# Alpha, key and query loaded as runs of three tokens, identity products in place of transposes, and POOL's order at gate piece 2

## What is computed

```python
# 1: gated linear attention; state starts at zero
for t in range(S):
    state = alpha[:, :, t, :, None] * state + einsum('bhd,bhe->bhde', k[:, :, t], v[:, :, t])
    y[:, :, t] = einsum('bhd,bhde->bhe', q[:, :, t], state)
x = y.transpose(0, 2, 1, 3).reshape(B * S, H * D)
# 2: normalised gated network, d_ff = 1536
xn = x / sqrt(mean(x * x, -1) + 1e-6) * rms_g
x = (silu(xn @ w_gate) * (xn @ w_val)) @ w_out
# 3: four experts of width 1024, weighted by normalised probabilities p
out = sum(p[:, e:e+1] * (relu(x @ w1[e]) @ w2[e]) for e in range(4))
```

## Time and profile before

| | us |
|---|---|
| median of 3 runs | 703.69 (703.68 to 704.35) |
| the profiled execution's own time | 704.28 |
| its span, first to last instruction | 702.2 |
| PE busy in it | 687.1 (98%) |
| DVE busy | 460.6 (66%) |
| POOL busy | 320.3 (46%) |
| ACT busy | 259.9 (37%) |

### The profile page before, as it was taken

How to read it: one execution, slowest core, us unless ns; L and a number is a source line. 1 busy time by engine, 2 the same in 40 slices (tenths; PEclk the granted TensorE clock), 3 DMA queues, 4 the chain that set the end, 5 groups by cost and what they waited for, 6 DMA issues and landing times.

```text
span 702.2 us, 10687 instructions
## 1 busy us (share of the span) xinstructions
PE 687.1 (98%) x3998; PEld 636.4 (91%) x3998; DVE 460.6 (66%) x808; ACT 259.9 (37%) x472; POOL 320.3 (46%) x401
## 2 busy tenths in 40 slices
PE   7889999999999999999999999999999999999998
PEld 6679999999999999998899999999999999999997
DVE  6975656655545633315848777877787779777876
ACT  3931234222522243226413344434343434443430
POOL 3467771111111124840294685558555865577200
PEclk9999999999999999999999999999999999999999
DMA  8994380005102000200001101110111001100003
GB/s 180 225 180 111 84 174 14 7 4 103 35 1 77 1 1 24 68 0 1 1 22 47 46 1 45 46 46 4 42 46 46 23 23 46 45 24 1 22 1 135
DMA packets 71749, 35.13 MB, mean 50 GB/s; under 512 B 53905, under 2 KB 70673, under 8 KB 71697
## 3 DMA queue, kind: packets, MB, share of 16 engines
q1 hardware_dynamic: 71696, 34.44, 19.5%
HBM read 31.48 MB, written 2.36 MB: 48 GB/s over the span
## 4 chain that ended last, share of the span: by engine, by line
PE 90%; SPq 6%; DVE 2%; issue 1%; POOL 1%; DMA 1%; ACT 0%; DVEq 0%
PE out_ps L1339 13%; PE out_ps L1341 13%; PE out_ps L1340 13%; PE hid_ps L1332 7%; PE hid_ps L1334 7%; PE hid_ps L1333 7%; PE at_ps L1544 4%; PE at_ps L1543 4%; PE at_ps L1542 4%; SPq L453 3%; PE hid_ps L1543 2%; PE hid_ps L1544 2%; PE hid_ps L1542 2%; PE at_ps L1382 2%; PE at_ps L1396 1%; PE at_ps L1428 1%
## 5 line engine op out<-in xcount | busy, mean ns | idle before, releaser
L1214 DVE SCALAR_TENSOR_TENSOR x<-out_ps,prob,x 128x384 f32<-128x384 f32 x180 | 110.3, 613 | 58.7 <-PE out_ps L1341 58.7
L1339 PE MATMUL out_ps<-early_r,late_r 128*128 128x384 f32 x384 | 129.1, 336 | 0.3 <-DVE x L1214 0.3
L1340 PE MATMUL out_ps<-early_r,late_r 128*128 128x384 f32 x384 | 129.4, 337 | 0.0
L1341 PE MATMUL out_ps<-early_r,late_r 128*128 128x384 f32 x384 | 129.3, 337 | 0.0
L669 POOL TENSOR_TENSOR hid_lo<-act_sb,hid_hi 128x384 fp32r<-128x384 f32 x44 | 45.0, 1022 | 170.3 <-ACT hid_hi L857 170.3
L913 ACT COPY late<-at_ps 128x512 f32<-128x512 f32 x98 | 57.7, 589 | 108.0 <-PE at_ps L1544 105.2
L1179 DVE TENSOR_TENSOR act_sb<-hid_ps,act_sb 128x384 f32<-128x384 f32 x48 | 26.6, 554 | 80.5 <-PE hid_ps L1334 71.1
L1339 PEld LDWEIGHTS out_ps<-early_r,late_r 128*128 128x128 f32 x384 | 72.1, 188 | 6.6 <-DVE x L1214 0.9
L1340 PEld LDWEIGHTS out_ps<-early_r,late_r 128*128 128x128 f32 x384 | 72.0, 188 | 5.3
L1341 PEld LDWEIGHTS out_ps<-early_r,late_r 128*128 128x128 f32 x384 | 72.1, 188 | 0.0
L723 POOL TENSOR_TENSOR early<-stage 128x128 f32<-128x128 f32 x14 | 6.5, 467 | 129.4 <-PE at_ps L1544 102.5
(11 more groups left out here) (272 smaller groups left out, 1614.5 us busy)
## 6 DMA issues: line engine op xcount, KB each, us to landing
stage<-in_moe_w_dram SPq DMA_DIRECT2D x32, 384.0 KB, 3.3
alpha_all<-in_alpha_dram SPq DMA_DIRECT2D x8, 288.0 KB, 6.1
stage<-in_moe_w_out_dram SPq DMA_DIRECT2D x4, 576.0 KB, 4.1
out_dram<-x SPq DMA_DIRECT2D x12, 192.0 KB, 1.9
stage<-in_moe_w_gate_dram SPq DMA_DIRECT2D x8, 216.0 KB, 4.1
stage<-in_moe_w_val_dram SPq DMA_DIRECT2D x8, 216.0 KB, 4.0
a_tm<-in_alpha_dram SPq DMA_DIRECT2D x9, 192.0 KB, 3.8
k_tm<-in_k_dram SPq DMA_DIRECT2D x9, 192.0 KB, 4.0
```

Of the source, the lines that this page charges most:

```text
L1214: dve.scalar_tensor_tensor(out=a, in0=part, scalar=p, in1=a, op0=ALU.mult, op1=ALU.add).then_inc(s_acc, 1)
L1339: pe.matmul(dst, ah, bh, start=first, stop=False)
L1340: pe.matmul(dst, ah, bl, start=False, stop=False)
L1341: return pe.matmul(dst, al, bh, start=False, stop=last)
```

## The change

The three tiles become [128, 8, 160]: a head's 160 columns are three tokens of 48 and one hole of 16 behind them. Partition p holds tokens 3p, 3p + 1 and 3p + 2, so a run in DRAM is 144 numbers, 576 bytes, and one DMA loads what three did. PE turns each head and token slot with one float32 product with the identity (64 columns of the head as the weights, 48 of the slot and 16 of what follows, the identity as the moving operand), whose 128 results go to every third column of the bank: 6 products for a tensor of a pair in place of 3 transposes. The semaphore counts follow (16 in place of 48), the clamp and the hole fill run over the smaller tiles. The value tensor keeps its three DMAs. On POOL, `hidden_lo(1)` moves from behind `split(3)` to a place inside it, after the rounding (L596) and before the wait for it and the subtractions.

```diff
+    HEAD = NCH * D + HOLE
-        q_tm = sb("q_tm", [P, NCH, H * LANE], stack=reg_a)
-        k_tm = sb("k_tm", [P, NCH, H * LANE], stack=reg_a)
-        a_tm = sb("a_tm", [P, NCH, H * LANE], stack=reg_a)
+        q_tm = sb("q_tm", [P, H, HEAD], stack=reg_a)
+        k_tm = sb("k_tm", [P, H, HEAD], stack=reg_a)
+        a_tm = sb("a_tm", [P, H, HEAD], stack=reg_a)
...
-                for c in range(NCH):
-                    sp.dma_start(dst[:, c, :].rearrange("p (h x) -> p h x", h=H)[:, hs, 0:D],
-                                 src[b, hs, t0 + c * CH:t0 + (c + 1) * CH, :].rearrange("h p d -> p h d")
-                                 ).then_inc(arrived or done, 16)
+                if which < 3:
+                    sp.dma_start(dst[:, hs, 0:NCH * D],
+                                 src[b, hs, t0:t0 + TQ, :].rearrange("h (p c) d -> p h (c d)", c=NCH)
+                                 ).then_inc(arrived or done, 16)
+                    return
...
-        def split(pool, n):
+        def split(pool, n, between=None):
...
             pool.tensor_scalar(hi, stage_view(n % 2, *shape), 0.0, 1.0, ALU.add, ALU.mult).then_inc(s_whi, 1)
+            if between:
+                between()
             pool.wait_ge(s_whi, n + 1)
...
-                make(pool.memset(t[:, :, :].rearrange("p c (h x) -> p (c h) x", h=H)[:, :, D:LANE], 1.0))
+                make(pool.memset(t[:, :, NCH * D:HEAD], 1.0))
...
-                    if f < FT - 1:
+                    if f < FT - 1 and FT * i + f != 1:
                         hidden_lo(FT * i + f)
                     if i == 0 and f < NPIECE - EARLY:
-                        split(pool, EARLY + f)
+                        split(pool, EARLY + f, None if f else lambda: hidden_lo(1))
...
-                        part = a_tm[:, :, 0:H // 2 * LANE] if f else a_tm[:, :, H // 2 * LANE:]
+                        part = a_tm[:, 0:H // 2, :] if f else a_tm[:, H // 2:, :]
...
                         for c in range(NCH):
-                            mm = pe.transpose(banks[bank][:, c * CH:(c + 1) * CH],
-                                              tm[:, c, n * 2 * LANE:(n + 1) * 2 * LANE], ident[:, :])
+                            for a in range(2):
+                                mm = pe.matmul(banks[bank][a * LANE:(a + 1) * LANE, bass.ds(c, CH, step=NCH)],
+                                               tm[:, 2 * n + a, c * D:c * D + LANE], ident[:, :], start=True,
+                                               stop=True)
```

More of the change, by code:

```diff
@@ L450, in load_quarter @@
                 hs = slice(first_head, last_head)
-                src, dst, done = ((alpha, a_tm, s_qka[0]), (k, k_tm, s_qka[1]), (q, q_tm, s_qka[2]), (v, v_tm, s_v))[which]
+                if which < 3:
+                    src, dst, done = ((alpha, a_tm, s_qka[0]), (k, k_tm, s_qka[1]), (q, q_tm, s_qka[2]))[which]
+                    sp.dma_start(dst[:, hs, 0:NCH * D],
+                                 src[b, hs, t0:t0 + TQ, :].rearrange("h (p c) d -> p h (c d)", c=NCH)
+                                 ).then_inc(arrived or done, 16)
+                    return
                 for c in range(NCH):
-                    sp.dma_start(dst[:, c, :].rearrange("p (h x) -> p h x", h=H)[:, hs, 0:D],
-                                 src[b, hs, t0 + c * CH:t0 + (c + 1) * CH, :].rearrange("h p d -> p h d")
-                                 ).then_inc(arrived or done, 16)
+                    sp.dma_start(v_tm[:, c, :].rearrange("p (h x) -> p h x", h=H)[:, hs, 0:D],
+                                 v[b, hs, t0 + c * CH:t0 + (c + 1) * CH, :].rearrange("h p d -> p h d")
+                                 ).then_inc(arrived or s_v, 16)
             def fill_holes(i):
@@ L1025, in _ @@
                     if i == 0:
-                        part = a_tm[:, :, 0:H // 2 * LANE] if f else a_tm[:, :, H // 2 * LANE:]
+                        part = a_tm[:, 0:H // 2, :] if f else a_tm[:, H // 2:, :]
                     if i == 0 and f == 0:
-                        dve.wait_ge(s_half[0], 16 * NCH)
+                        dve.wait_ge(s_half[0], 16)
                     else:
-                        dve.wait_ge(s_qka[0], 16 * NCH * (i + 1))
+                        dve.wait_ge(s_qka[0], 16 * (i + 1))
                     dve.tensor_scalar(part, part, MID - HALF, MID + HALF, ALU.max, ALU.min).then_inc(s_clamp, 1)
@@ L1366, in _ @@
                         if which and i == 0 and f < 2:
-                            pe.wait_ge(s_half[which], 16 * NCH)
+                            pe.wait_ge(s_half[which], 16)
                         elif which:
-                            pe.wait_ge(s_qka[which], 16 * NCH * (i + 1))
+                            pe.wait_ge(s_qka[which], 16 * (i + 1))
                         else:
```

## The result

| | before | after |
|---|---|---|
| median of the runs of the comparison, us | 703.68 (703.14 to 704.35) | 714.20 (713.58 to 714.94) |
| the profiled execution's own time | 704.28 | 714.69 |
| its span | 702.2 | 712.6 |

The changed kernel is slower: the ratio is 1.0159, with a 95% interval of 1.0137 to 1.0181. Forecast were 716.5, in a range of 710 to 735. The forecast was right in the signs of its terms and in the places where they fall; its largest term was 1.6 to 1.9 us too large.

A forecast was written before the change was run, and what follows sets the result against it. PE was taken to be full from 57 to 250 us, so instructions added there lengthen the run. Products +18.4, value products -1.7, wait -4.1 and start +0.2 sum to +12.8 us, giving 716.5 us, range 710 to 735.

The forecast's parts named there:

- The products: PE's turning in quarters 1 to 3: twelve pairs with products at 0.066 us each instead of transposes, +18.4 us.
- the lower bound: PE's product spacing if the two halves overlap perfectly: half of a transpose's 0.109, 0.0545 us, making the products +13.5 us.
- The value products: PE in quarters 1 to 3: later arrival ends the waits for DVE at nine slow value products, -1.7 us.
- The wait: PE's wait for hidden_lo at 50.5 to 53 us: 2.4 us and the slow clock behind it go, -4.1 us.
- twice, counts once: Either POOL's swap or the new loads alone would remove PE's wait for hidden_lo; the -4.1 us counts once.
- The start: Quarter 0's attention alone, where DVE and ACT bound: later scans against less DMA and a shorter clamp, +0.2 us.
- the weight pieces' earlier landing: At the first G, which waits for DVE and ACT, not weights: claimed to be worth nothing.
- Queue-bound start: Rival: the start hangs on SP's DMA queue, so all 6.2 us freed there come off, 710.1 us; chance 8%.
- loads pace the start: Rival: quarter 0's stage moves with its DMA packets, 11.1 us goes, 705.2 us; chance 8%.
- The halves don't overlap: Rival: PE's two half-width products don't run beside each other, 0.109 us each, +31.4, 735.1 us; chance 12%.
- The stepped output costs: Rival: PE results to every third column double the spacing to 0.132 us, +41.3, 745.0 us; chance 9%.
- The wait stays: Rival: no earlier hidden_lo(1), 4.1 us less gained, 720.6 us; within the forecast's own range, whose chance is 63%.

The follow-up runs named there:

- t_and_tq_together: The changed kernel with query's turning placed right behind that of alpha and key, one block of 18 products instead of two: 711.08 us, ratio 1.0114.
- transposes_on_runs: The changed kernel with three full-width transposes per tensor in place of six products, turning the wrong columns at the same counts: 699.99 us, ratio 0.9956.
- swap_only: The kernel before with POOL's new order alone, loads and transposes as they were: 700.65 us, ratio 0.9970.
- no_swap: The changed kernel with POOL's old order, hidden_lo(1) behind the whole split of piece 3: 714.94 us, ratio 1.0168.
- swap_piece4: The kernel before with POOL's new order and weight piece 4 loaded ahead of quarter 1's values: 701.50 us, ratio 0.9966.
- products_only: The kernel before, old loads and POOL order kept, each transpose replaced by two 64-lane products writing neighbouring columns: 716.59 us, ratio 1.0197.
- halves_in_turn: The changed kernel with a tensor's three lower-half products first, then its three upper-half ones: 720.56 us (one execution).

## Why the prediction was right, step by step

**The products** (+18.4; measured 16.5, 16.8 with the first pair's T). The mechanism was right, the size was off by one number. TQ and AHEAD give the spacing: (2.12 - 0.81)/24 = 0.0546, half of a transpose's 0.109, so the halves overlap perfectly and the lower bound was the truth for the spacing. What is left of TQ, 0.81 - 12 x 0.0546 = 0.155, is paid once on entry into half-width products. My 0.066 came from L1428, whose 0.79 for 12 contains such an entry: 0.79 - 0.155 is 0.053 each, and in the trace of before its instructions start in pairs every 0.109. TQ, a block of 12 like L1428's, came out as forecast (0.79, measured 0.81); T and AHEAD, two and three times as long, did not (1.58 and 2.38, measured 1.31 and 2.12). Had I taken the row apart so, I would have charged the entry once per block and not per product. T has no entry (24 x 0.0546 = 1.31) since L1438, half-width itself, stands in front of it. The exit I took as 0.15 is 0.20. So two terms were missized on opposite sides: 36 x 0.066 = 2.38 where 2.12 was paid, and 0.30 of exits where it was 0.40. t_and_tq_together shows the exit by itself, and half of the entry.

**The value products** (-1.7). The 0.39 of 79.91 is 0.17 in the changed kernel, and none of the nine is left: as forecast. That the later PE is the reason is borne out by transposes_on_runs, which has the new loads and the short turning: there all nine stand again (0.38 to 0.40 six times, 0.32 to 0.33 three times).

**The wait** (-4.1; measured 4.2 between the profiled executions). Right, and "twice, counts once" as well: swap_only and no_swap each take it away. The size hangs on the execution of the kernel before: the 4.1 was read from one, and over 23 of them swap_only gains 2.1. The low part of piece 3 was ready at 52.43 (forecast 52.5) and G 3 came at 54.07; split(4) ended at 56.59 (56.7) and V 3 began at 58.57 (58.5). Here the longer turning helps: without it and with the old loads, in swap_only, PE is early enough for piece 4 to be 0.27 late.

**The start** (+0.2; measured +0.07). That it came out near is luck, for it is not made of the parts that I named. PE's timeline and DVE's, in the changed kernel:

```profile
1.12 4.63 PE L1354 MATMUL hid_ps<-ones 128*128 128x128 f32 x20 [1.12 <-DVE ones L1026]
5.69 1.21 PE L1391 MATMUL at_ps<-ident,a_tm 128*64 128x128 f32 x12
...
6.95 1.05 DVE L1045 TENSOR_TENSOR_SCAN dec<-at_ps,zero 128x128 f32<-128x128 f32 x3 [2.37 <-PE at_ps L1391]
...
33.67 0.56 DVE L1117 TENSOR_TENSOR x_nrm<-x_raw 128x384 f32<-128x384 f32 x1
```

Alpha was clamped by 4.58, but the warm-up ran to 5.75 (4.63 us, where rows 8 have 4.29), and the first block's 12 products took 1.04 to the start of the next (6.73) where the loop's spacing makes 0.66. The first scan is 0.71 late (6.95 for 6.24), and 27 us later DVE still is: its square of x starts at 33.67 instead of 32.95. There it is won back, not by PE. Before, the same square and POOL's work beside it were

```profile
32.95 1.41 DVE L1109 TENSOR_TENSOR x_nrm<-x_raw 128x384 f32<-128x384 f32 x1
...
33.90 1.33 POOL L601 TENSOR_TENSOR wvl<-stage,wvh 128x384 fp32r<-128x384 f32 x1
```

1.41 with POOL splitting a weight piece at the same time, 0.56 in the changed kernel, where POOL had finished that piece by 30.2 since the weights landed earlier. I had called the weight pieces' earlier landing worth nothing there, and that step was wrong: it was worth 0.85 us through POOL's company, not through PE's wait. That the two engines slow each other is borne out by the other runs, though none was made for it: the same square takes 0.56 in all six kernels with the new loads, where POOL is idle beside it, and 0.79, 0.81 and 0.88 in swap_piece4, swap_only and products_only, where POOL subtracts; how much it loses differs.

**The rivals.** *Queue-bound start* and *loads pace the start* fell with transposes_on_runs: with the new loads and cheap turning G 1 is 0.5 earlier, not 6 or 11. *The halves don't overlap* fell with the 0.0546. *The stepped output costs* fell twice: 1.31 stepped and 1.31 in products_only, 0.98 stepped in transposes_on_runs and 0.98 before. The Trainium skill's rule on non-contiguous access patterns (PSUM — Partial Sum Buffer, "Specifications (TRN2)") is not borne out for float32 results at a step of three. *The wait stays* fell: PE's list of waits has none for POOL's `hidden_lo`.

## What to carry to other kernels

Where PE is full, count its instructions before anything else: 25,000 DMA packets fewer and the new order on POOL were together worth 4.3 us between profiled executions (3.1 over the runs), about the worth of one wait, and half-width products in place of full-width transposes cost 16.8 with both halves of the array fully overlapped, because a transpose is one instruction of 0.109 and the two float32 products in its place are four of 0.055, with an entry and an exit for each block on top. When a price is taken from a neighbouring row, take its entry and exit apart from its spacing first, by two blocks of different length. And a gap of 2.4 us on PE, once seen in the list of waits, is best closed by the smallest edit that closes it: here the reordering of one POOL step alone, 0.9970 (0.9954 to 0.9987), beats both kernels. What such a wait is worth is read from many executions of the kernel that has it, not from one.

## What the runs showed of the hardware

- The two column halves take their instructions independently: 0.0546 us per float32 instruction of 128 columns with both busy, 0.109 with one, and the halves may be at different tensors (the last two in halves_in_turn).
- Going from full-width to half-width products costs 0.155 us, and back 0.20, once per block of 12 to 36 instructions.
- A gap on PE can cost more than itself, when the granted clock falls behind it: 2.4 us of waiting and 1.7 of slow products in the profile before. In products_only and swap_piece4 gaps of 1.0 and 0.9 us were followed by no fall. The same gaps don't always do the same: around 12 and 14 us PE has waits of 0.67 and 0.60 us both before and in swap_only, and the clock over 10 to 20 us is 1.00 before and 0.83 there.
- In one comparison the kernel before varied from 700.44 to 705.73 us in 23 runs, swap_only from 700.12 to 702.65 in 12. Of the 23, the four with a mean granted clock of 1.000 took 700.44 to 701.54, the two with 0.993 took 704.46 and 705.73. A wait and a fall of the clock that are not of the same length each time would fit that spread; it is not shown, as the profile is of one execution.
